# Opening of an FFT, mixing and two-layer feed-forward kernel: another layout of x, another order of early loads and late tiles, and one store in halves

## What is computed

```python
X = np.fft.rfft(x, axis=1)                       # x: 2 x 3008 x 256, f32
Yr = Xr @ w_r - Xi @ w_i + b_r
Yi = Xr @ w_i + Xi @ w_r + b_i
Y  = softshrink(Yr, 0.01) + 1j * softshrink(Yi, 0.01)
y  = np.fft.irfft(Y, n=3008, axis=1)             # 6016 tokens of 256
h = y @ moe_w_in;   g = max(h, 0) + alpha * min(h, 0);        z = g @ moe_w_out
h = z @ moe2_w_in;  g = h if h >= 1, 0 if h <= -1, else (h + 1)**2 / 4;  out = g @ moe2_w_out
```

## Time and profile before

| | |
|---|---|
| median of three runs | 1205.69 us (1203.91 to 1211.31) |
| the profiled execution, whole | 1203.19 us |
| its span, first to last instruction | 1201.2 us |
| start of the first `real47` matmul | 7.09 us |
| start of `forward(0)` | 35.62 us |
| mean granted clock of TensorE | 0.993 |

### The profile page before, as it was taken

The page is one execution under the profiler, slowest core; times in us unless marked ns, Lnnn a source line. Parts: engine busy times, 40 slices in busy tenths (PEclk is TensorE's granted clock), DMA queues, the critical chain, the costliest instruction groups (busy, mean ns, idle before and its releaser), DMA issues.

```text
span 1201.2 us, 21026 instructions
## 1 busy us (share of the span) xinstructions
PE 1173.2 (98%) x6944; PEld 1136.2 (95%) x6944; DVE 883.6 (74%) x1681; ACT 850.4 (71%) x1874; POOL 683.0 (57%) x714
## 2 busy tenths in 40 slices
PE   7899989999999999999999999999999999999997
PEld 2689979999999999999999999999999999999997
DVE  2577777777777777777777777777778787878765
ACT  2335547777777777767667788888878787878775
POOL 0005645766675757766566666565757575757543
PEclk9899999999999999999999999999999999999999
DMA  9677720212102111112004510101010101000001
GB/s 292 197 240 233 230 87 1 67 57 63 40 28 83 42 62 41 53 57 76 19 2 146 182 59 1 27 1 27 1 27 1 25 3 22 6 17 11 12 16 27
DMA packets 63748, 77.47 MB, mean 64 GB/s; under 512 B 31156, under 2 KB 43572, under 8 KB 63636
## 3 DMA queue, kind: packets, MB, share of 16 engines
q1 hardware_dynamic: 60156, 69.45, 19.2%
q10 hardware_dynamic: 3484, 6.68, 1.6%
HBM read 45.83 MB, written 30.28 MB: 63 GB/s over the span
## 4 chain that ended last, share of the span: by engine, by line
PE 92%; POOL 3%; DMA 1%; ACT 1%; DVE 1%; issue 1%; SPq 0%; POOLq 0%; DVEq 0%; ACTq 0%
PE bank L1120 78%; PE bank L1087 6%; PE bank L1106 2%; PE bank L1063 2%; POOL g_lo L502 2%; PE bank L1074 2%; PE bank L1097 2%; DMA slots_scratch<-a_sb 1%; POOL prep_raw L528 0%; DMA x_sb<-x 0%; POOL xc_lo L477 0%; DMA zt<-slots_scratch 0%; ACT g_hi L744 0%; POOL prep_raw L513 0%; ACT prep_hi L767 0%
## 5 line engine op out<-in xcount | busy, mean ns | idle before, releaser
L502 POOL TENSOR_TENSOR g_lo<-g_sb,g_hi 128x376 fp32r<-128x376 f32 x510 | 505.2, 1002 | 374.0 <-ACT g_hi L744 373.4
L1120 PE MATMUL bank<-g_hi,w_out_hi 128*128 128x376 f32 x1024 | 344.9, 337 | 0.8 <-POOL g_lo L502 0.4
L1120 PE MATMUL bank<-g_lo,w_out_hi 128*128 128x376 f32 x1024 | 342.0, 334 | 0.0
L1120 PE MATMUL bank<-g_hi,w_out_lo 128*128 128x376 f32 x1024 | 341.7, 334 | 0.0
L1120 PE MATMUL bank<-xc_hi,w_in_hi 128*128 128x376 f32 x896 | 302.3, 337 | 0.6 <-DVE partial L900 0.2
L1120 PE MATMUL bank<-xc_hi,w_in_lo 128*128 128x376 f32 x896 | 300.3, 335 | 0.0
L1120 PE MATMUL bank<-xc_lo,w_in_hi 128*128 128x376 f32 x896 | 298.5, 333 | 0.0
L744 ACT ACTIVATE g_hi<-g_sb 128x376 fp32r<-128x376 f32 x512 | 261.1, 510 | 44.2 <-DVE g_sb L937 28.6
L1120 PEld LDWEIGHTS bank<-g_hi,w_out_hi 128*128 128x128 f32 x1024 | 192.4, 188 | 8.8 <-POOL g_lo L502 7.4
L1120 PEld LDWEIGHTS bank<-g_hi,w_out_lo 128*128 128x128 f32 x1024 | 192.4, 188 | 0.0
L1120 PEld LDWEIGHTS bank<-g_lo,w_out_hi 128*128 128x128 f32 x1024 | 192.3, 188 | 0.0
(11 more groups left out here) (77 smaller groups left out, 1524.7 us busy)
## 6 DMA issues: line engine op xcount, KB each, us to landing
gc<-group_consts SPq DMA_DIRECT2D x24, 256.0 KB, 4.2
slots_scratch<-a_sb ACTq DMA_DIRECT2D x16, 384.0 KB, 5.1
zt<-slots_scratch SPq DMA_DIRECT2D x24, 256.0 KB, 3.9
inverse_scratch<-v_sb SPq DMA_DIRECT2D x24, 256.0 KB, 3.1
ut<-inverse_scratch SPq DMA_DIRECT2D x16, 384.0 KB, 4.9
x_sb<-x SPq DMA_DIRECT2D x16, 320.0 KB
prep_raw<-wpack SPq DMA_DIRECT2D x16, 256.0 KB, 2.6
out<-yt SPq DMA_DIRECT2D x120, 32.0 KB, 1.6
```

What stands on the lines that cost most here:

```text
L502: pool.tensor_tensor(g_lo[kind][:, :], g_sb[n % 3][:, :], g_hi[kind][:, :].bitcast(f32), ALU.subtract)\
L1120: done = pe.matmul(out_ap, w, g, start=first and n == 0, stop=last_one and n == 2, skip_group_check=unchecked)
```

## The change

The host lays x out as 16 tiles of 96 x 1024, each in one piece and with its two padding rows as zeros. A tile is then loaded by one DMA, the padding DMAs and their semaphores are gone, and tile 0 comes in two halves of 512 columns, the matrix between them; PE's first matmul waits for the first half alone. SP's order is another: the mixing weights, the first group matrices and the bias stand among the first loads, and tile 10 is loaded once tile 6 has been computed. The store of tile 7, the last of batch 0, is made in two halves: ACT stores the left one as soon as it has copied it, SP stores the right one. ACT splits the mixing weights after tile 8, DVE after tile 9. Tile 11 stays in step 1, and tiles 12 to 15 go to steps 4, 7, 10 and 13; their loads are issued at other places of SP's loop. The number of tiles ahead of the first step is 11 in both.

```diff
-LATE_TILES = {1: FIRST_TILES, 7: FIRST_TILES + 1, 10: FIRST_TILES + 2, 13: FIRST_TILES + 3, 16: FIRST_TILES + 4}
+LATE_TILES = {1: FIRST_TILES, 4: FIRST_TILES + 1, 7: FIRST_TILES + 2, 10: FIRST_TILES + 3, 13: FIRST_TILES + 4}
+LATE_LOADS = {4: FIRST_TILES + 2, 5: FIRST_TILES + 3, 7: FIRST_TILES + 4}
+HALF_COLS = TILE_COLS // 2
...
             def load_x(t):
-                for lo, hi in ((0, 80), (80, ROWS)):
-                    q = t % TILES_PER_BATCH
-                    sp.dma_start(x_sb[lo:hi, t, :],
-                                 x_rows[t // TILES_PER_BATCH, lo:hi, q * TILE_COLS:(q + 1) * TILE_COLS])\
-                      .then_inc(x_in[t], 16)
+                sp.dma_start(x_tile(t), x[t, :, :]).then_inc(x_in[t], 16)
...
-            for t in range(FIRST_TILES):
+            sp.dma_start(x_tile(0)[:, 0:HALF_COLS], x[0, :, 0:HALF_COLS]).then_inc(x_half_in, 16)
+            sp.dma_start(fwd_sb[:, :], fwd47).then_inc(fwd_in, 16)
+            sp.dma_start(x_tile(0)[:, HALF_COLS:], x[0, :, HALF_COLS:]).then_inc(x_in[0], 16)
+            for t in range(1, TILES_PER_BATCH + 1):
                 load_x(t)
-                if t % TILES_PER_BATCH == 0:
-                    b = t // TILES_PER_BATCH
-                    if b == 0:
-                        sp.dma_start(fwd_sb[:, :], fwd47).then_inc(fwd_in, 16)
-                    sp.dma_start(x_sb[ROWS:ROWS_PAD, t:t + TILES_PER_BATCH, :].rearrange("p t c -> p (t c)"),
-                                 x_rows[b, 0:ROWS_PAD - ROWS, :]).then_inc(pad_in[b], 16)
+            sp.dma_start(wm_raw[:, :], wmix).then_inc(wm_in, 16)
             load_matrices(0)
-            sp.wait_ge(a_done, 2 * (TILES_PER_BATCH + 1))
-            sp.dma_start(wm_raw[:, :], wmix).then_inc(wm_in, 16)
-            sp.wait_ge(a_stored[0], 16 * TILES_PER_BATCH)
+            load_x(TILES_PER_BATCH + 1)
+            sp.dma_start(bias_sb[:, :], bias).then_inc(bias_in, 16)
+            sp.wait_ge(a_done, 2 * (TILES_PER_BATCH - 1))
+            load_x(TILES_PER_BATCH + 2)
+            t = TILES_PER_BATCH - 1
+            sp.wait_ge(a_right, t + 1)
+            sp.dma_start(az_rows[0, 0:ROWS_PAD, t * TILE_COLS + HALF_COLS:(t + 1) * TILE_COLS],
+                         a_tile(t)[:, HALF_COLS:]).then_inc(a_stored[0], 16)
+            sp.wait_ge(a_stored[0], 16 * (TILES_PER_BATCH + 1))
             load_values(0)
-            sp.dma_start(bias_sb[:, :], bias).then_inc(bias_in, 16)
             load_x(FIRST_TILES)
...
                 load_values(p)
                 load_matrices(p)
+                if p in LATE_LOADS:
+                    load_x(LATE_LOADS[p])
                 store_pair(p - SLOTS)
...
             def store_a(t):
                 b, q = t // TILES_PER_BATCH, t % TILES_PER_BATCH
                 act.wait_ge(a_left, t + 1)
+                if t == TILES_PER_BATCH - 1:
+                    act.dma_start(az_rows[b, 0:ROWS_PAD, q * TILE_COLS:q * TILE_COLS + HALF_COLS],
+                                  a_tile(t)[:, 0:HALF_COLS]).then_inc(a_stored[b], 16)
+                    return
                 act.wait_ge(a_right, t + 1)
...
             def real47(t, banks):
-                pe.wait_ge(x_in[t], 32)
-                if t % TILES_PER_BATCH == 0:
-                    pe.wait_ge(pad_in[t // TILES_PER_BATCH], 16)
                 for part, copied in enumerate((a_left, a_right)):
+                    if t == 0 and part == 0:
+                        pe.wait_ge(x_half_in, 16)
+                    else:
+                        pe.wait_ge(x_in[t], 16)
...
+    tiles = np.zeros((TILES, ROWS_PAD, TILE_COLS), x.dtype)
+    tiles[:, :ROWS] = x.reshape(BATCH, ROWS, TILES_PER_BATCH, TILE_COLS).transpose(0, 2, 1, 3)\
+                       .reshape(TILES, ROWS, TILE_COLS)
```

More of the change, by code:

```diff
@@ L208, in fft_mix_ffn_kernel @@
         x_in = [sem(f"x_in{i}") for i in range(TILES)]
-        pad_in = [sem(f"pad_in{i}") for i in range(BATCH)]
+        x_half_in = sem("x_half_in")
         a_done = sem("a_done")
@@ L364, in _ @@
                 load_matrices(p)
-            sp.wait_ge(b_done, 3)
-            for t in range(FIRST_TILES + 1, FIRST_TILES + 3):
-                load_x(t)
+            load_x(FIRST_TILES + 1)
+            sp.dma_start(alpha_sb[:, :], alpha).then_inc(const_in, 16)
+            sp.dma_start(inv47[:, :], inv_in).then_inc(const_in, 16)
             for p in range(SLOTS, PAIRS):
[L370 to L373, removed]
                 if p == PAIRS // 2:
@@ L571, in copy_a @@
                 act.wait_ge(a_done, 2 * t + 1)
-                act.activation(a_tile(t)[:, 0:512], bank_a[0:ROWS_PAD, :], ACT.Copy).then_inc(a_left, 1)
+                act.activation(a_tile(t)[:, 0:HALF_COLS], bank_a[0:ROWS_PAD, :], ACT.Copy).then_inc(a_left, 1)
             def store_a(t):
@@ L583, in _ @@
                 store_a(t)
-            act.wait_ge(wm_in, 16)
-            act.activation(wm_hi[:, :], wm_raw[:, :], ACT.Copy).then_inc(wm_hi_ready, 1)
+                if t == TILES_PER_BATCH:
+                    act.wait_ge(wm_in, 16)
+                    act.activation(wm_hi[:, :], wm_raw[:, :], ACT.Copy).then_inc(wm_hi_ready, 1)
             def split_xt(s):
@@ L810, in copy_a @@
                 dve.wait_ge(a_done, 2 * t + 2)
-                dve.tensor_copy(a_tile(t)[:, 512:1024], bank_a[0:ROWS_PAD, :]).then_inc(a_right, 1)
+                dve.tensor_copy(a_tile(t)[:, HALF_COLS:], bank_a[0:ROWS_PAD, :]).then_inc(a_right, 1)
             for t in range(FIRST_TILES):
                 copy_a(t, a_bank[(2 * t + 1) % 4])
-            dve.wait_ge(wm_hi_ready, 1)
-            dve.tensor_tensor(wm_lo[:, :], wm_raw[:, :], wm_hi[:, :].bitcast(f32), ALU.subtract)\
-               .then_inc(wm_lo_ready, 1)
+                if t == TILES_PER_BATCH + 1:
+                    dve.wait_ge(wm_hi_ready, 1)
+                    dve.tensor_tensor(wm_lo[:, :], wm_raw[:, :], wm_hi[:, :].bitcast(f32), ALU.subtract)\
+                       .then_inc(wm_lo_ready, 1)
             def split_xt(s):
@@ L1056, in real47 @@
             def real47(t, banks):
-                pe.wait_ge(x_in[t], 32)
-                if t % TILES_PER_BATCH == 0:
-                    pe.wait_ge(pad_in[t // TILES_PER_BATCH], 16)
                 for part, copied in enumerate((a_left, a_right)):
+                    if t == 0 and part == 0:
+                        pe.wait_ge(x_half_in, 16)
+                    else:
+                        pe.wait_ge(x_in[t], 16)
                     if t >= 2:
                         pe.wait_ge(copied, t - 1 if t < FIRST_TILES else t)
-                    pe.matmul(banks[part][0:ROWS_PAD, :], fwd_sb[:, :], x_tile(t)[:, part * 512:(part + 1) * 512],
+                    pe.matmul(banks[part][0:ROWS_PAD, :], fwd_sb[:, :], x_tile(t)[:, part * HALF_COLS:(part + 1) * HALF_COLS],
                               start=True, stop=True).then_inc(a_done, 1)
@@ L1262 @@
     arrays = {
-        "x": x,
+        "x": tiles,
         "wmix": np.concatenate([columns(w_r), columns(w_i)], axis=1),
```

3 lines of the change are left out of this document (removed).

## The result

The changed kernel took 1200.51 us in the median of eleven executions against 1207.48 us for the kernel before in the same series. One of the eleven took 2325.57 us, nearly twice as long as the others, for no reason that the record shows, and the ratio leaves it out. The ratio is 0.9948, with a 95% interval of 0.9934 to 0.9961: 6.3 us less, where the two medians alone give 7.0. Timed again in a later series it came to 0.9963 (0.9947 to 0.998), 4.5 us less. So the change makes the kernel 0.4 to 0.5% faster, some 5 us. Both intervals exclude 1, but the gain is less than the 1% that the prediction gives as the least clear difference. I had forecast 0.9% with a range of 1191.5 to 1202.

The account below looks back on a forecast made before the run. PE was taken as busy 98% of the span, so time is won only where it idles or runs at lower clock: -7.6 - 3.55 + 0.4 = -10.75 us, forecast 1195.0 us, 0.9% less, range 1191.5 to 1202.

Parts of the forecast that it names:

- Start, 3.0 us earlier: First matmul at 4.05 us, waiting only for half of tile 0 and the matrix; 3.0 us earlier, bounds 2.5 and 3.5.
- Do the later loads keep up? Yes, by either rate.: Opening tiles: PE needs one per 1.72 us; even at 253 GB/s a tile loads in 1.55 us.
- x at 365 GB/s in the new layout: Opening loads: contiguous x priced at 365 GB/s, 11.9 us for eleven tiles, against 17 before.
- Store landed at 24.2: Tile 7's halves, last stores of batch 0, land at 24.2 us; before, the store landed at 31.8.
- rival C: x read no faster in its new layout: stores land about 28.3, forward(0) at 32.1, low clock, 1202.2 us; chance 0.13.
- B: Stores land at 25.2 to 26.5 us, PE idles over 3.5 us, clock falls; 1199.5 to 1200.7 us; chance 0.21.
- D: Slower than before: right half of tile 7's store crowded out on SP's queue; about 1208 us; chance 0.04.
- Forward(0) at 28.0, and the clock kept: After the first read back: forward(0) 7.6 us earlier; clock holds, so first forward matmuls, tile 11 and mix save 3.55 us.
- Tile 11, 0.4 us: Step 1: waiting for tile 11's load, issued right behind the read back, charged 0.4 us, bounds 0 and 0.8.
- Late tiles and the splits on ACT and DVE at nothing: Moved late tiles cost PE 1.72 us in any step; splitting mixing weights earlier delays nothing needed; 0 us.

Follow-up runs that it names:

- layout_only: The kernel before with x laid out by tiles, one DMA a tile, no padding DMAs, order of loads, stores and late tiles unchanged; ratio to before 0.9984.
- x_2k: The changed kernel with each tile of x laid out as two blocks of 96 x 512, moved in 2 KB rows; ratio to before 0.9945.
- fillers: The changed kernel with unread matmuls where PE waits, ahead of tiles 9, 10, forward(0) and tile 11; ratio to before 0.9960.
- x11_early: The changed kernel with tile 11 loaded ahead of the wait for the stores and of the first read back; ratio to before 0.9955.
- late_back: The changed kernel with tiles 12 to 15 back in steps 7, 10, 13 and 16; ratio to before 0.9961.
- wm_behind: The changed kernel with mixing weights and bias issued behind SP's half of tile 7's store, weights split after tile 10; ratio to before 0.9954.
- Reordered: The paced kernel with weights and bias behind the first read back, 2 KB rows of x, four unread matmuls ahead of forward(0); ratio to before 0.9985.
- whole_store: The changed kernel with tile 7 stored whole by ACT when both copies are done; ratio to before 0.9958.
- paced: As wm_behind, and SP issues tiles 5 to 10 one by one, tile t once tile t - 4 is computed; ratio to before 0.9960.
- a_again: The changed kernel without edit, for a second profile; ratio to before 0.9963, span 1199.9 us.

## Why the prediction came out as it did

The sign, the range and "within 1%" were right, but the size was about twice the measured one: 10.7 us of gain forecast, 4.5 to 6.3 us measured. That the time fell into the range is in part luck, since the mechanism was not the forecast one.

The two first profiles differ by 2.2 us in the start of mix(1) (43.80 and 41.63), and the terms of the sum can be read off them. Forward(0) came 3.4 us earlier, where 7.6 were forecast. The work that the clock was to speed up, the first forward matmuls, tile 11 and mix(0), took 0.4 us less (7.21 for 7.58), where 3.55 were forecast. The wait for tile 11 cost 1.6 us, where 0.4 were charged. Point by point:

*Start, 3.0 us earlier.* It was 3.8 us (7.09 to 3.32), outside the bounds of 2.5 and 3.5. Right in kind, a little short, because the matrix landed in 2.1 us and not in 2.9. Only 2.6 us of it reached tile 7 in this pair of profiles, since PE ran longer at its slow start (17.22 us for the eight tiles, 16.07 before).

*"Do the later loads keep up? Yes, by either rate."* Wrong. I had compared PE's pace with the rate of x alone. Once the stores begin, the two share 416 GB/s, and tile 9, behind the weights, the matrices and eight tiles, was the first to miss its time (17.3 us to landing).

*x at 365 GB/s in the new layout.* This is the step that failed first. For a share of one, layout_only gives 244 GB/s for contiguous tiles (251/1.03), the changed kernel 262 to 268 and x_2k 265, against 250 before. I had taken the rate of reads from 636 us on, at a share of 0.91, for the rate of a contiguous read; the difference was not the layout. The 5 us that this should have saved were the bulk of the earlier landing. Why the reads at 636 us are faster stays open: they fill 128 partitions, not 96, and come from a tensor that the kernel itself has written, and no run tried either.

*Store landed at 24.2.* Measured 28.85 and 28.02: 3 to 4.5 us earlier than before, not 7.6. The rival C had named this case, with a landing at 28.3 and the low clock, at 1202.2 us, just outside the range. By the prediction's own sum it should have been 29.3 (24.2 and the 5.1 us that x then costs more). It is C that the traces show. The measured 1200.5 lies in the numbers of B, 1199.5 to 1200.7, but the stores landed after B's 25.2 to 26.5 us, so that is chance. D did not come true in full, though the half on SP's queue was the last to land.

*Forward(0) at 28.0, and the clock kept.* It came at 32.23 and 30.87, late because the stores were; the read back itself took 3.3 and 2.8 us and not 3.75. The clock fell in the opening in every profile without fillers, at times already while PE waited for tile 9. I had priced it at 3.55 us. In fillers, at a clock of 1.00, the forward matmuls (eight, not four), tile 11 and mix(0) took 1.16, 1.94 and 1.45 us, 3.0 us less than before. So the price was about right for this work, but the whole kernel was no faster than the changed one: the gain in these blocks did not reach the time, or is too small to tell.

*Tile 11, 0.4 us.* It was 1.6 us in the trace (load landed 5.66 us after its issue). x11_early removed the pause and gained nothing.

*Late tiles and the splits on ACT and DVE at nothing.* Right for the tiles: the part from mix(1) on takes the same time in the two first profiles, and late_back is not distinguishable. Right for the weights too, as far as wm_behind shows: with them behind the last store the ratio is the changed kernel's. Reordered shows that they cost time when they come behind the read back. In the kernel before they were split by 33.7 us, ahead of forward(0), so the change had nothing to gain there. The sum priced the weights for the last store alone and not for tiles 9 and 10, which stood behind them.

What the measured gain is made of can be said only in part. The layout with the padding gone is worth about 2 us (0.9984). The rest, about 3 us, comes with the other edits. Late_back, whole_store and wm_behind each took one of them back, the places of the late tiles, the halves of tile 7 and the early weights, and each kept 0.9954 to 0.9961, so that none of the three is needed by itself. The start by half a tile (PE at 3.3 us, not 4.9 as in layout_only), the later load of tile 10 and the order of SP's loads behind the first read back were not run one by one, so the cause of these 3 us stays open. The traces do not contradict the timed runs: mix(1) is at 44.4 us in the mean of two profiles of before and at 40.8 of two after, 3.6 us apart.

## What to carry to other kernels

Where a stage is held by the DMA engines, price each wait by the bytes that must be through before it, at the rate with reads and writes together, and do it for every consumer, not only for the last one. A saturated queue moves a gain rather than paying it: sooner stores came back as a slower read back, and a sooner read back as later weights. Take the rate of a transfer from a row in which the same mix of traffic runs, and measure an edit of a few tenths of a per cent by repeated timing, since two profiles of the same kernel differed by 1.0 and 2.3 us in their span here.

## What the runs showed of the hardware

In this opening, over windows of 8 to 13 us, reads of DRAM with nothing beside them ran at 244 to 268 GB/s for a DMA share of one, whether rows were 4 KB with a step of 32 KB (before), 4 KB in one piece (layout_only, after) or 2 KB in one piece (x_2k). With stores beside them the same engines moved 387 to 416 GB/s at shares of 1.01 to 1.04. So a share of one does not tell that the engines move as much as they can.

A store that ACT issues while SP's queue is full of reads can stand still for 5 us. In the changed kernel the first was issued at 7.86 us, and q10 shows no packet until 13.0; in the kernel before it was issued at 11.61, with no packet until after 16.5. They landed 8.2 and 8.3 us after their issue. In paced, where SP held loads back, q10 moved from 11 us on for an issue at 7.90. For that time the reads ran alone, at the lower rate.

The Trainium skill has a rule that bears on the layout: the page "DMA: Bandwidth & Descriptors", section "Latency and other measured facts", reports lower rates for rows with a large power-of-two pitch and advises padding the pitch or contiguous tiles. The smallest pitch in its figures is 512 KiB; at the 32 KB of this kernel no run showed a difference (250 against 244 to 268 GB/s).

The clock: the same eight tiles took 15.88 to 17.97 us over the profiles in which PE did not wait among them, with the same instructions, by how long the matmuls kept the 0.86 us of the start. The granted clock reads 1.00 in that stretch, so that this slow start shows in durations only.

The granted clock fell to 0.50, 1.2 GHz, not only in the 7.3 us wait of the kernel before. In the changed kernel PE waited 2.6 us, worked for 1.16 and waited again, and the clock fell at 33.7 us, 0.35 us into that second wait. It can also fall when PE is at work again: in wm_behind at 24.3 us, 1.6 us after a wait of 1.65 us had ended, and in a_again at 151.7 us, 1.8 us after one of 2.4 us. In wm_behind the same wait of 2.4 us near 148 us left it at 2.4 GHz.
